# Attention, mixture of experts and a Mish feed-forward part in one kernel: other places and times for the expert weights, logits by quarters of the tokens, M in two steps

## The reference

```python
# attention, 16 heads; a query sees the keys of its own hash bucket (6 bits)
bits = (q @ proj > 0)                      # the same for k
scores = where(q_bucket == k_bucket, q @ k.T / 8, -1e9)
x = softmax(scores) @ v                    # -> [1536, 512]
# soft mixture of 8 experts with 4 slots each
logits = x @ phi                           # [1536, 32]
d = exp(logits - logits.max(0)); d /= d.sum(0) + 1e-9      # over the tokens
slot_input = d.T @ x                       # [32, 512]
slot_out[e] = relu(slot_input[e] @ w1[e]) @ w2[e]          # w1 [512, 1024], w2 [1024, 512]
c = softmax(logits, axis=1)
x = c @ slot_out                           # [1536, 512]
# feed-forward part
h = x @ w_in                               # [1536, 2048]
out = (h * tanh(softplus(h))) @ w_out      # Mish
```

## Time and profile before

| | us |
|---|---|
| the profiled execution, device time | 528.01 |
| its span, first to last instruction | 526.2 |
| three timed runs | 529.7, 534.05, 534.4 |
| median of the three | 534.05 |
| mean granted TensorE clock (1 is 2.4 GHz) | 0.963 |
| PE busy | 463.2 (88%) |
| DVE busy | 307.0 (58%) |
| ACT busy | 305.7 (58%) |
| POOL busy | 127.1 (24%) |

### The profile page before, as it was taken

The page is one execution under the profiler, slowest core; times in us unless marked ns, Lnnn a source line. Parts: engine busy times, 40 slices in busy tenths (PEclk is TensorE's granted clock), DMA queues, the critical chain, the costliest instruction groups (busy, mean ns, idle before and its releaser), DMA issues.

```text
span 526.2 us, 7349 instructions
## 1 busy us (share of the span) xinstructions
PE 463.2 (88%) x2658; PEld 310.0 (59%) x2658; DVE 307.0 (58%) x500; ACT 305.7 (58%) x465; POOL 127.1 (24%) x83
## 2 busy tenths in 40 slices
PE   4479999999999999999877785675997989999996
PEld 3356676766666676666433222132776868877874
DVE  5255656556555656666254111069999888888840
ACT  2378787887878787877350100027465666676750
POOL 3040303040301303000000000061444545544450
PEclk9799999999999999999997987798899999999999
DMA  8896747798578854760094999920000020002002
GB/s 194 170 213 147 163 98 152 202 314 172 121 153 303 207 130 87 188 256 1 14 401 187 353 397 396 386 103 1 1 0 0 1 80 1 0 0 80 0 1 80
DMA packets 49328, 75.67 MB, mean 144 GB/s; under 512 B 24752, under 2 KB 27696, under 8 KB 48688
## 3 DMA queue, kind: packets, MB, share of 16 engines
q1 hardware_dynamic: 48792, 73.85, 47.8%
q10 hardware_dynamic: 504, 1.39, 1.1%
HBM read 51.45 MB, written 3.15 MB: 104 GB/s over the span
## 4 chain that ended last, share of the span: by engine, by line
PE 74%; DVE 9%; DMA 8%; issue 4%; ACT 3%; POOL 1%; ACTq 0%; DVEq 0%; POOLq 0%
PE unit L304 32%; PE o_acc L304 24%; PE unit L933 13%; DMA w<-in_moe_w 6%; DVE fu L833 2%; PE o_acc L899 2%; DVE g L844 2%; DVE fe L828 1%; PE o_acc L961 1%; PE unit L1004 1%; DVE nmax L710 1%; DMA op<-bit 1%; POOL g_lo L528 1%; ACT fe L647 1%; DMA turned<-in_q 1%
## 5 line engine op out<-in xcount | busy, mean ns | idle before, releaser
L710 DVE TENSOR_REDUCE nmax<-unit 128x1 f32<-128x768 f32 x96 | 91.8, 956 | 89.1 <-PE unit L304 88.2
L563 ACT ACTIVATE probs<-unit,shift,keep 128x768 f32<-128x768 f32 x96 | 95.5, 995 | 54.0 <-DVE shift L713 54.0
L304 PE MATMUL unit<-op 128*128 128x512 f32 (+1 forms) x384 | 92.5, 363 | 6.5 <-DMA op<-bit 6.5
L528 POOL TENSOR_TENSOR g_lo<-g,g_hi 128x1024 fp32r<-128x1024 f32 x24 | 73.1, 3047 | 88.3 <-ACT g_hi L654 88.3
L933 PE MATMUL unit<-ident,probs 128*128 128x128 f32 x576 | 81.7, 278 | 5.3 <-ACT probs L563 5.1
L933 PEld LDWEIGHTS unit<-ident,probs 128*128 128x128 f32 x576 | 62.5, 140 | 39.3 <-ACT probs L563 23.3
L572 ACT COPY turned<-unit 128x768 f32<-128x768 f32 x96 | 76.5, 797 | 0.3 <-PE unit L933 0.3
L304 PE MATMUL o_acc<-turned,vn 128*64 128x384 f32 x384 | 72.1, 498 | 0.0
L304 PEld LDWEIGHTS unit<-op 128*128 128x128 f32 x384 | 59.1, 192 | 15.8 <-issue 11.1
L304 PE MATMUL unit<-wo_hi,g_hi 128*128 128x512 f32 x96 | 38.9, 405 | 12.4 <-DVE m_pack L822 5.5
L844 DVE TENSOR_TENSOR g<-fv,fr 128x1024 f32<-128x1024 f32 x24 | 46.0, 1915 | 3.8 <-ACT fr L663 3.8
(11 more groups left out here) (123 smaller groups left out, 595.1 us busy)
## 6 DMA issues: line engine op xcount, KB each, us to landing
w<-in_moe_w SPq DMA_DIRECT2D x16, 2048.0 KB, 11.4
op<-cuts SPq DMA_DIRECT2D x31, 384.0 KB
op<-cuts SPq DMA_DIRECT2D x31, 192.0 KB
w_in_sb<-in_moe_w_in SPq DMA_DIRECT2D x1, 4096.0 KB, 18.0
wo_raw<-in_moe_w_out SPq DMA_DIRECT2D x2, 2048.0 KB, 17.9
vn<-in_v SPq DMA_DIRECT2D x8, 384.0 KB, 3.2
out_x<-stage SPq DMA_DIRECT2D x12, 256.0 KB, 2.4
qn<-in_q SPq DMA_DIRECT2D x14, 192.0 KB, 4.1
```

Of the source, the lines that this page charges most:

```text
L304: return nc.tensor.matmul(out_, lhsT, rhs, start=start, stop=stop, skip_group_check=True)
L528: gp.tensor_tensor(g_lo[n % 2][:, :], g[n % 2][:, :], g_hi[n % 2][:, :].bitcast(F32), ALU.subtract).then_inc(g_lo_done, 1)
L563: sc.activation(probs[i % 3][:, :], unit("S", i)[:, 0:S], ACT.Exp, bias=shift[:, g % 4, t:t + 1], scale=keep[:, g % 4, t:t + 1], accum_out ...
L710: ve.tensor_reduce(nm, unit("S", i)[:, 0:S], AX.X, ALU.max, negate=True).then_inc(max_done, 1)
```

## The change

- **Places for the weights.** The scratch area ahead of the first tile is set to 512 bytes for each partition instead of 16,384 (`dynamic_dma_scratch_size`). w2 gets a fourth place. `load_w2(2)` is issued behind `load_w1(3)`, before `normed`; `load_w2(3)` takes its position behind `normed`, ahead of w_in. The fifth w1 place moves over `xT`, so w1(4) waits for `logits_done` instead of `si_done`. The order behind it: w1(5), w2(4), w2(5), w1(6), w1(7), w2(6), w2(7), and the halves of w_out.
- **Logits by quarters.** 16 matmuls of 32 columns of the array and 384 tokens: each quarter of the tokens has its 32 partitions of one bank, and the width is added up in the bank. Maximum, Exp and copy then work on 128 x 384. Each quarter has a maximum and a sum of its own; dT isn't normalized before it is turned: the slot inputs are scaled instead, by a factor that puts the four quarters together (`fit_row`, `d_fit`, `d_part`, `d_den`, `d_scale`: small operations and three small PE operations, two of them between the slot-input matmuls). Transposes are 3 + 3 of 128 x 128 and one of a column. Two bank clears move ahead of the logits. The part for c (maximum over the slots, Exp, sums) stands behind the copy of the slot inputs on DVE.
- **M in two steps.** `so_t` is copied once. `m_shares(n)`: four matmuls side by side in 32 columns of the array each; ACT copies them (`m_part`); `make_m(n)` is one matmul that adds them and writes the four copies. The steps of the first token block are written out in another order on ACT, DVE and PE, with the second piece of `cut_w_out` at step 2.
- **g_lo.** In all blocks PE runs 16 of the 24 output matmuls after `g_hi`, and waits for `g_lo` only before the last 8.
- **First head.** ACT makes the high part of k, DVE the rest (also the low part of q, which was POOL's). SP waits until all eight transfers of head 0 have landed before it issues the constants and transfers of head 1.

```diff
-        top = [16512]
+        top = [SCRATCH + 128]
...
+        w2_sb = [sb(f"w2_{n}", [P, FC, DM], at=[a]) for n, a in enumerate(
+            (ring_at + W1, ring_at + SLOT + W1, third_at, third_at - W1))]
+        W1_PLACE, W2_PLACE = (0, 1, 2, 3, 4, 0, 1, 3), (0, 1, 2, 3, 0, 1, 2, 3)
...
             spread_bits(sp, 0, 0)
+
+            done, count = ops_of(0)
+            sp.wait_ge(done, count)
             sp.wait_ge(const_rows, 1)
...
             load_w1(3)
+            load_w2(2)
 
             sp.wait_ge(normed, G)
-            load_w2(2)
+            load_w2(3)
             sp.dma_start(w_in_sb[:, :, :], w_in.rearrange("(c p) f -> p c f", p=P)).then_inc(w_in_in, 16)
-            sp.wait_ge(si_done, 1)
+            sp.wait_ge(logits_done, 1)
             load_w1(4)
 
-            for layer, e in ((1, 5), (2, 3), (2, 4), (1, 6), (2, 5), (1, 7), (2, 6), (2, 7)):
+            for layer, e in ((1, 5), (2, 4), (2, 5), (1, 6), (1, 7), (2, 6), (2, 7)):
...
             copy_turned(1)
+            act.wait_ge(t_copied, 2)
+            act.wait_ge(hi_done, 1)
+            sc.copy(cuts[:, 2, :], qk_t[:, 1, :]).then_inc(hi_done, 1)
             spread_key_parts(act, 0)
...
+            for c in range(C):
+                for b in range(4):
+                    ins = mm(banks[4][NS * b:NS * b + NS, 0:LW], phi_sb[:, c, :], xT[:, c, LW * b:LW * (b + 1)], c == 0,
+                             c == C - 1)
+            ins.then_inc(logits_done, 1)
...
+            def m_shares(n):
+                for c in range(C):
+                    ins = mm(m_psum[n][NS * c:NS * c + NS, :], so_t[:, c, :], w_in_sb[:, c, n * 512:(n + 1) * 512], True)
+                ins.then_inc(parts_done, 1)
...
+                pe.wait_ge(g_hi_done, nth(t, NUN, n))
...
+                        mm(out_psum[o], g_hi[n % 2][:, a], wo_hi[:, w, :], start, False)
+                        mm(out_psum[o], g_hi[n % 2][:, a], wo_lo[w // 8][:, w % 8, :], False, False)
+                pe.wait_ge(g_lo_done, nth(t, NUN, n))
+                for f in range(2):
+                    for o in range(4):
...
+                        ins = mm(out_psum[o], g_lo[n % 2][:, a], wo_hi[:, 2 * n + f, :], False, n == NUN - 1 and f == 1)
```

More of the change, by code:

```diff
@@ L16 @@
 MISH_TOP = 4.851651954097903e8
+SCRATCH = 512
 def build_program(nc, q, k, v, proj, phi, w1, w2, w_in, w_out, out):
@@ new lines, in copy_high, with exponent, cut_high @@
+            def copy_high(n):
+                act.wait_ge(hw_done, n + 1)
+                sc.copy(m_hi[:, 512 * n:512 * (n + 1)], m_psum[n]).then_inc(mhi_copied, 1)
+            def exponent(t, n):
+                act.wait_ge(h_done, nth(t, NUN, n))
+                if again(t, n):
+                    act.wait_ge(u_done, nth(t, NUN, n - 2))
+                sc.activation(fe[n % 2][:, :], h_psum(n % 2), ACT.Exp).then_inc(e_done, 1)
+            def cut_high(t, n):
+                act.wait_ge(g_done, nth(t, NUN, n))
+                if again(t, n):
+                    act.wait_ge(out_done, nth(t, NUN, n - 2))
+                sc.copy(g_hi[n % 2][:, :], g[n % 2][:, :]).then_inc(g_hi_done, 1)
@@ L662, in ff_step @@
[L662 to L663 removed]
+                    invert(*at)
                 at = lagged(j, u, 3, NUN)
```

394 lines of the change are left out of this document (216 added, 178 removed).

## The result

Four executions of the changed kernel took 509.77 to 513.29 us, median 511.47, beside 529.7 to 534.4, median 534.01, of the kernel before on the same chip: ratio 0.961, 95% interval 0.955 to 0.966. The forecast was 513.0. The profiled execution took 509.77 us, its span is 507.9 where it was 526.2, so the traces have 18.3 us to account for; the sum of the terms was 19.1. The forecast of 513 stood between 508.9 (the sum off the profile) and 514.9 (off the median), so part of its closeness is the choice of that base.

A forecast was written before the change was run, and what follows sets the result against it. PE bounds attention and the last two token blocks, weight DMA the expert stage, DVE the first token block. Terms 2.2 + 12.5 + 1.2 + 3.2 = 19.1 us gave 508.9 off the profile, 514.9 off the median; forecast 513, range 504 to 521.

The forecast's parts named there:

- Weights: Expert stage, waiting for weights: closed DMA hole (7.2) and one unit fewer (5.3) gain 12.5 us, bounds 9 and 15.
- the hole closes (7.2): DMA queue in the expert stage: w1(4), issued at 269.9 while w_in flows, removes a 7.2 us standstill.
- the rival of the dry queue: Expert stage: cold PE and small operations delay w1(5) to 285 or later; stage gives 9, total time 517.5; chance 0.14.
- Start: First head: scores at 17.0 instead of 19.89; gain 2.2 us at the attention's end, bounds -1 and 3.5.
- I take 0.7: Start-up: SP's wait delays head 1's transfers, needed by DVE's `bits` of pair 1; 0 to 2.4 us given back, 0.7 taken.
- M: From `so_t` to M's first rounded part: 4.48 us becomes about 3.3; 1.2 us counts, bounds 0 and 2.
- First token block: First token block, where PE waited for DVE's chain: 3.2 us gained beyond M, bounds 0 and 6.
- hide `g_lo`: 3.1: First token block: the first 16 output matmuls need only `g_hi`, complete at 400.6 against 403.73, saving 3.1 us.
- the new order ... can shift by 2 us either way: First token block: which DVE operations meet POOL's `g_lo` and are stretched can shift by 2 us either way.
- That the transfers need the scratch: DMA scratch cut: its cost was taken as zero but kept among rivals; sign, SP's issues growing everywhere; no chance given.
- Head 1 late: Start-up: SP's issues take the full 11 us and `bits` blocks the maximum; start gives nothing, 516 us; chance 0.08.
- DVE keeping the block: First token block: DVE's sum is unchanged, only M's 1.2 counts and PE goes cold; 517 us; chance 0.12.

The follow-up runs named there:

- w1_late: The changed kernel with w1(4) issued only when the slot inputs are done, as before the change; 510.89 us, ratio 0.964.
- logits_blocks: The changed kernel with logits, maxima, Exp and slot inputs of the kernel before (three blocks of 512 tokens); 518.12 us, ratio 0.975.
- w2_late: The changed kernel with w2(2) issued behind `normed`, ahead of w2(3), as before the change; 513.83 us, ratio 0.968.
- warm_start: The changed kernel plus 28 transposes of the identity, read by nothing, on PE ahead of the first scores; 512.49 us, ratio 0.966.
- old_order: The changed kernel with the first token block's order of the kernel before on ACT, DVE and PE, M still in two steps; 514.82 us, ratio 0.971.
- all_three: The changed kernel plus transposes ahead of first scores and last pair's second-layer matmuls, and output copies ahead of `g` at block boundaries; 507.34 us, ratio 0.957.
- m_one_step: The changed kernel with each quarter of M made by four matmuls over a fourfold `so_t`, new order kept; 514.33 us, ratio 0.971.
- before_split: The kernel before with one edit: PE waits for `g_lo` only before the last 8 of 24 output matmuls; 530.13 us, ratio 1.000.
- lo_first: The changed kernel with PE waiting for `g_lo` before all 24 output matmuls again; 512.27 us, ratio 0.966.
- no_head_wait: The changed kernel without SP's wait for head 0's transfers to land; 513.03 us, ratio 0.966.
- warm_w2: The changed kernel plus 28 unread transposes on PE between the last pair's first-layer and second-layer matmuls; 510.81 us, ratio 0.964.
- stage_first: The changed kernel with DVE's copies of the output block ahead of the next block's `g` at each boundary; 508.50 us, ratio 0.960.

## Why the prediction was right, and where its steps were not

**Weights, 12.5 forecast, 12.7 measured** between the two profiles, 10.5 to 13.4 by all of them. The size within that spread, the place of the remaining hole and the condition (w1(5)'s release by `hid_done`) held. In the reason one step was wrong: "w1(4) is issued at the end of the logits ... the hole closes (7.2)". It closes as well with w1(4) released by the slot inputs (w1_late); what closes it is that `hid_done` comes 7 us earlier behind the attention, 21.85 us for 28.81, by the shorter softmax (logits_blocks, 5.4 to 7.6 us). The unit taken out from behind `normed`, 5.3 forecast, is 1.9 to 4.15 by w2_late. The chain ran without a clock fall in this profile and still ended at 281.5, where 280.4 follows from my terms with the start as measured: the slot inputs with the two small matmuls between took 3.7 us (271.43 to 275.10), not 2.9, and from there to `hid_done` it was 6.4, not 5.9. It can also run cold: in warm_start's profile the first pair's 32 matmuls took 5.10 us, `hid` came at 283.5, and the last w2 matmuls 65.6 us behind the attention. The profiles with such a cold chain (this one, old_order, all_three) have 65.2 to 65.6 there, those with a warm one 63.4 to 65.2. That is the rival of the dry queue, at 2.2 us or less of its 3.5.

The Trainium skill, DMA: Bandwidth & Descriptors, section "Anatomy of one DMA — SWDGE (gpsimd) path", gives 2.0 us + bytes at 436 GB/s for a DMA that GpSimd issues (those here are SP's), by which I had estimated a gain of 16 to 17. The full queue moved 413 GB/s in 272 to 278 us, 410 in 300 to 305 and 381 over the whole stage: by these a 2.10 MB unit is 5.1 to 5.5 us, nearer to the 5.3 of the rows of before than to the page's 4.8, and the measurement decides against the estimate.

**Start, 2.2 forecast, 1.1 measured** between a warm start and a cold one; 2.15 cold against cold, 1.4 to 1.6 warm against warm. First scores 17.40 for 17.0: ACT's two bit issues took 2.78 us beside SP's (12.55 to 15.33), not 1.6, so they ended 1.1 us later than forecast; the landing came 2.07 behind them, as forecast. (The text's own terms, 14.2 and 2, make 16.2 and not its 17.0.) What is given back behind the first scores, "I take 0.7", was 1.36 here, but in this profile by the cold PE, which the sum didn't have, and not by the mechanism that the text names. That mechanism is seen in the warm profiles: head 1 lands at 28.7 to 28.8 and `bits` waits 2.8 us for it, so that 0.8 to 0.9 us of the first scores' gain of 2.3 to 2.4 don't reach the end of the attention: about the 0.7 of the forecast. There both the first scores and this landing must come earlier for more to be gained.

**M, 1.2 forecast, 1.1 measured** to the first rounded part. But M in two steps is worth 3 us at output step 5 (m_one_step): the sum looked at the first pack only, and the second, 2.5 us earlier, is what the full DVE waits for. In the sum this hides in the next term.

**First token block, 3.2 forecast, 5.4 measured, 2.1 given back.** Wrong in two steps that cancel in part. "Now the first 16 matmuls ... hide `g_lo`: 3.1" is right inside the block (3.04 in before_split) and worth nothing at the end of the kernel, for "in the other blocks ... nothing" fails: they begin with DVE's copies behind DVE's `g`, and a PE that arrives earlier waits there longer, 2.87 us for 1.69, and slower afterwards. And "the new order ... can shift by 2 us either way" undervalued the order, which with M's second step gives 3.4. What reached the end from M and this block is 4.5 us, where 4.4 was forecast; since the missed steps cancel, the agreement is largely luck.

**Rivals.** That the transfers need the scratch is out: SP's four issues take 4.10 us where they took 4.16, and the expert stage moves 381 GB/s. So the statement in the Trainium skill, SBUF — State Buffer, section "SBUF size: 192, 224, or 256?", that the carveout is the ring of software-made descriptors, agrees with this trace. The agreement says no more than that these DMAs don't need the 16 KiB. Head 1 late is true in part: it takes 0.8 to 0.9 us of the gain where PE is warm. DVE keeping the block is false. The totals of the rivals (517.5, 517, 516, 508) don't follow from one base: off the 532.1 that the forecast of 513 implies they are 516.5, 516.2, 515.2 and 509.1, and the 546 is 544.

## What to carry to other kernels

Before a wait is priced, look at what its engine meets next: here 2.5 of 3 us saved in one block were lost from the first hand-over on, until the engine that hands over did its copies first. Where a queue of transfers has a hole, find which release ends the hole, and change that one alone; an earlier issue in front of it changed nothing. Of two things that end within a microsecond of each other, speeding up one shows only the other. And before two profiles are subtracted, see from the durations of like matmuls whether PE was warm in both.

## What was not expected of the hardware

- Warm matmuls in one place made the next stage cold: with transposes in the 4 us wait the last 32 matmuls ran in 3.62 us for 5.47, and `so_t` to `m_hi` took 5.01 for 3.36 (4.87 in all_three). In w2_late, lo_first, no_head_wait and logits_blocks M was cold without them. What decides it isn't known from these runs.
- After a wait of 2.75 to 2.87 us at the block boundary the granted clock fell to 0.50 within 2 us and was back some 4 us behind the wait's end (404.5 to 408.5 in the changed kernel); after 1.13 to 1.72 us at the same place it stayed at 1.00, in each of the six profiles read there (before, w2_late, lo_first, warm_w2, stage_first, all_three).
- DVE's `fu` took 3.29 us where it began while POOL's `g_lo` ran and 1.23 us where it began a quarter to half a us before it (w2_late, stage_first); which meets which depended on the order of DVE's copies.
- The column of the granted clock can miss a slow stretch at the start: it says 1.00 from 14 to 30 us in before_split and no_head_wait, whose four score matmuls take 1.63 us there, as in the changed kernel at 0.50, where they take 0.95 in the kernel before at 1.00.
